# Attention of a fused kernel rewritten in unit slots: V and ones stationary, softmax weights moving, operands stacked by DMAs, convolution on VectorE

## What is computed

```python
# attention: a key counts only where the 6-bit hash of q and k agrees
q_bits = (q @ proj) > 0; k_bits = (k @ proj) > 0      # buckets of 6 bits
mask = q_bucket[:, None] == k_bucket[None, :]
scores = where(mask, scale * q @ k.T, -1e9)
attn = exp(scores - max(scores)); attn /= sum(attn) + 1e-9
x = attn @ v                                          # 16 heads of 768x768
# gated convolution
gate = sigmoid(causal depthwise convolution of x, 5 taps)
y = (gate * (x @ w_val)) @ w_out
# Fourier mixing and feed-forward
u = y + real(fft(fft(y, axis=1), axis=2))
out = u + relu(norm(u) @ w_ch1) @ w_ch2
```

## Time and profile before

| what | value |
|---|---|
| device time, median of 3 runs | 797.1 us (795.99 to 800.96) |
| span of the profiled execution | 798.6 us |
| PE busy | 746.9 us, 94% |
| PEld busy | 704.5 us, 88% |
| DVE busy | 389.7 us, 49% |
| ACT busy | 271.1 us, 34% |
| POOL busy | 352.6 us, 44% |
| DMA | 29.13 MB, mean 36 GB/s |

### The profile page before, as it was taken

One profiled execution on the slowest core, in us unless ns is written; L12 is line 12 of the kernel. 1 busy time (PEld: TensorE's weight loads), 2 busy tenths in 40 slices (PEclk: granted clock), 3 DMA queues, 4 the chain that ended last, 5 costly groups with the idle time before them and its releaser, 6 DMA issues.

```text
span 798.6 us, 12617 instructions
## 1 busy us (share of the span) xinstructions
PE 746.9 (94%) x4358; PEld 704.5 (88%) x4358; DVE 389.7 (49%) x680; ACT 271.1 (34%) x489; POOL 352.6 (44%) x334
## 2 busy tenths in 40 slices
PE   3898989899898889989999999999999999999998
PEld 2898988899798889989989899999999989999997
DVE  6655666655655765664476457953222212122112
ACT  4353534545245554524643343411111111111110
POOL 1237475574756657474987579578300000000000
PEclk9798978979889998979999999999999999999999
DMA  6010111111011111001012111333010001001001
GB/s 151 12 47 10 38 47 47 46 46 26 20 46 46 46 46 46 17 1 32 1 37 57 34 53 41 93 87 99 27 39 0 0 0 39 0 0 40 0 1 40
DMA packets 27938, 29.13 MB, mean 36 GB/s; under 512 B 14848, under 2 KB 19200, under 8 KB 27904
## 3 DMA queue, kind: packets, MB, share of 16 engines
q1 hardware_dynamic: 27904, 28.68, 13.0%
HBM read 25.52 MB, written 3.15 MB: 36 GB/s over the span
## 4 chain that ended last, share of the span: by engine, by line
PE 75%; DVE 13%; issue 5%; POOL 4%; ACT 1%; DMA 0%; SPq 0%; DVEq 0%; ACTq 0%; POOLq 0%
PE psum L1031 63%; PE psum L1082 9%; DVE a2k L770 3%; DVE a1q L768 3%; DVE max_half L783 2%; DVE den L806 2%; POOL taps L464 1%; ACT probs L599 1%; PE psum L1098 1%; PE psum L1107 1%; PE psum L1229 1%; DVE neg_parts L794 1%; DMA k_raw<-in_k 0%; PE psum L1088 0%; DVE neg_rest L796 0%
## 5 line engine op out<-in xcount | busy, mean ns | idle before, releaser
L1082 PEld LDWEIGHTS psum<-va,probs 128*128 128x128 f32 x1152 | 153.9, 205 | 6.0 <-ACT probs L599 4.3
L1082 PE MATMUL psum<-va,probs 128*128 128x65 f32 x1152 | 152.6, 284 | 3.2 <-ACT probs L599 3.2
L783 DVE TENSOR_REDUCE max_half<-psum 128x1 f32<-128x384 f32 x192 | 97.0, 551 | 82.0 <-PE psum L1031 79.8
L599 ACT ACTIVATE probs<-psum 128x384 f32<-128x384 f32 x192 | 86.0, 490 | 134.6 <-PE psum L1031 132.9
L1002 DVE SCALAR_TENSOR_TENSOR h_lo<-psum,h_hi 128x384 fp32r<-128x384 f32 x64 | 35.7, 558 | 183.3 <-ACT h_hi L749 183.3
L749 ACT ACTIVATE h_hi<-psum 128x384 fp32r<-128x384 f32 x64 | 31.5, 492 | 215.4 <-PE psum L1031 215.4
L1031 PE MATMUL psum<-a1k,a1q 128*128 128x384 f32 x192 | 78.9, 411 | 23.2 <-DVE max_half L783 20.2
L1031 PE MATMUL psum<-unt_hi,w_hi 128*128 (+1 forms) x256 | 86.9, 339 | 0.0
L1031 PE MATMUL psum<-unt_lo,w_hi 128*128 (+1 forms) x256 | 86.3, 337 | 0.0
L1031 PE MATMUL psum<-unt_hi,w_lo 128*128 (+1 forms) x256 | 85.9, 336 | 0.0
L1031 PE MATMUL psum<-a1q,a1k 128*128 128x384 f32 x192 | 75.1, 391 | 2.1 <-DVE a2q L777 1.9
(11 more groups left out here) (132 smaller groups left out, 1446.9 us busy)
## 6 DMA issues: line engine op xcount, KB each, us to landing
stg_w<-in_w SPq DMA_DIRECT2D x32, 256.0 KB, 2.6
k_raw<-in_k SPq DMA_DIRECT2D x32, 192.0 KB, 3.6
q_raw<-in_q SPq DMA_DIRECT2D x16, 192.0 KB, 3.3
va<-in_v SPq DMA_DIRECT2D x16, 192.0 KB, 3.1
out<-y SPq DMA_DIRECT2D x12, 256.0 KB, 2.1
stg_b<-in_w_b SPq DMA_DIRECT2D x16, 137.0 KB, 2.1
stg_a<-in_w_a SPq DMA_DIRECT2D x16, 128.0 KB, 2.7
proj_raw<-in_proj SPq DMA_DIRECT2D x1, 128.0 KB, 2.1
```

Of the source, the lines that this page charges most:

```text
L599: act.activation(probs[:, at_:at_ + HALF], psum[:, ST_BANKS[m % 2], 0:HALF], ACT.Exp, scale=SCALE).then_inc(exp_done, 1)
L783: dve.tensor_reduce(max_half[:, m:m + 1], psum[:, S_BANKS[m % 3], 0:HALF], AX.X, ALU.max).then_inc(max_done, 1)
L1082: mm = pe.matmul(psum[:, PV_BANK, t * DV:(t + 1) * DV], probs[:, at_:at_ + P], va3[par][:, j, :], start=(j == 0 and t == 0), stop=(j == T ...
```

## The change

All engines now follow one list of unit slots g, from -20 to 95 (and a few behind it), written out with no loop. A slot is one tile of 128 keys or queries with all 768 columns. On TensorE, slot g holds the turned scores of unit g+2, the scores of unit g+10, and `weigh_v` of unit g. Six slots are a head, twelve a pair.

- **`weigh_v`** loads the 128x128 block `v1` (64 columns of V, 64 of ones) as the weight and moves the 768 columns of `probs` past it in two float32 matmuls, of 384 and 385 columns. The result is already channels by queries, with the row sums beside it. The 385th column, of ones, gives the sum of all V, so L1088, `sum_v` and `turn_x` are gone.
- **`scores`** has one pair of banks instead of three single ones: it waits for the maximum of the unit directly before. `maximum` takes 768 columns in one instruction.
- **Stacking.** ScalarE and VectorE make hi and lo of q and k together (`hi_qk`, `lo_qk`, one instruction of 128x768 each per head), and six DMAs per head (`stack`) copy them from SBUF to SBUF into `a1q`, `a1k`, `a2q`, `a2k`. Hash bits of a pair of heads are made by one instruction and stacked by four DMAs (`stack_bits`). The hash of a pair is 12 matmuls at slot 10 of 12.
- **Rows of one number per query** are spread over partitions through memory: a flag row (no match) is stored and loaded back to 128 partitions (`spread_flag`), the denominators go to 128x6 (`fold_den`), their reciprocals are stored and loaded back to 64 partitions (`spread_rec`). Where a load follows a store, SP itself waits for the store.
- **VectorE** adds the flag's share and evacuates PSUM (`take_sums`) and computes the whole convolution, one instruction of 768 columns per tap. **GpSimd** keeps `split_weights` and multiplies with the reciprocal (`scale_x`).

```diff
-                for t in tiles:
-                    at_ = (j % 3) * S + t * P
-                    mm = pe.matmul(psum[:, PV_BANK, t * DV:(t + 1) * DV], probs[:, at_:at_ + P], va3[par][:, j, :],
-                                   start=(j == 0 and t == 0), stop=(j == T - 1), skip_group_check=True)
...
+                if j == 0:
+                    pe.wait_ge(v_loaded[par], 16 * (n // 2 + 1))
+                    if n > 0:
+                        pe.wait_ge(sums_ready, n)
+                pe.wait_ge(probs_ready, i + 1)
+                pe.matmul(first, v1[par][:, w], probs[i % PBUF][:, 0:HALF], start=j == 0, stop=j == T - 1)
+                pe.matmul(last, v1[par][:, w], probs[i % PBUF][:, HALF:PCOLS], start=j == 0, stop=j == T - 1).then_inc(pv_done, 1)
...
+            for g in range(FIRST, UNITS):
+                pair, n = g // (2 * T), g // T
+                if g % T == 3 and 0 <= n + 1 < NH:
+                    turn_max(n + 1)
+                if 0 <= g + ST_LEAD < UNITS:
+                    turned_scores(g + ST_LEAD)
+                if 0 <= g + S_LEAD < UNITS:
+                    scores(g + S_LEAD)
+                if g % (2 * T) == 10 and 0 <= pair + 2 < NPAIR:
+                    hash_pair(pair + 2)
+                if 0 <= g:
+                    weigh_v(g)
```

On SP (`stack` has two more copies of lo behind a wait for `qk_lo_ready`):

```diff
+                sp.dma_start(bits(a1q[s][0:D, :]), hi[0:D, :]).then_inc(set_loaded[s], 16)
+                sp.dma_start(bits(a1k[s][0:D, :]), hi[D:P, :]).then_inc(set_loaded[s], 16)
+                sp.dma_start(bits(a1k[s][D:P, :]), hi[D:P, :]).then_inc(set_loaded[s], 16)
+                sp.dma_start(bits(a2q[s][0:D, :]), hi[0:D, :]).then_inc(set_loaded[s], 16)
...
+                sp.wait_ge(max_rows, n + 1)
+                sp.dma_start(flag_dram[n:n + 1, :], bits(a2q[n % SETS][FLAG:FLAG + 1, :])).then_inc(flag_stored, 16)
+                if n >= 2:
+                    sp.wait_ge(sums_ready, n - 1)
+                sp.wait_ge(flag_stored, 16 * (n + 1))
+                sp.dma_start(flag_b[n % 2][:, :], flag_dram[n:n + 1, :].to_broadcast([P, S])).then_inc(flag_loaded[n % 2], 16)
...
+                if g % (2 * T) == 10 and 0 <= pair + 3 < NPAIR and pair + 3 >= RAWS // 2:
+                    load_qk(2 * (pair + 3))
+                    load_qk(2 * (pair + 3) + 1)
+                if g % (2 * T) == 6 and 0 <= pair + 2 < NPAIR:
+                    stack(2 * (pair + 2))
+                if g % (2 * T) == 10 and 0 <= pair + 2 < NPAIR:
+                    stack(2 * (pair + 2) + 1)
+                if g % (2 * T) == 0 and 0 <= pair + 1 < NPAIR:
+                    stack_bits(pair + 1)
```

More of the change, by code:

```diff
@@ L502, in fold_tile @@
+            for g in range(FIRST, UNITS + T):
+                n = g // T
+                if g % T == 1 and 0 <= n < NH:
+                    split_weights(n)
+                if g % T == 4 and 1 <= n <= NH:
+                    scale_x(n - 1)
+                    pool.wait_ge(x_ready, n)
             def fold_tile(b, f):
@@ new lines, in lo_x @@
+            def lo_x(b, c):
+                at_ = (CT * b + c) * S
+                dve.wait_ge(x_hi_ready, CT * b + c + 1)
+                dve.tensor_tensor(x_lo[:, c * S:(c + 1) * S], xT[:, at_:at_ + S], bits(x_hi[:, c * S:(c + 1) * S]), ALU.subtract).then_inc(x_lo_ready, 1)
+            dve.wait_ge(conv_loaded, 16)
+            for g in range(FIRST, UNITS):
+                pair, n = g // (2 * T), g // T
+                if g % T == 0 and 1 <= n:
+                    take_sums(n - 1)
+                if 0 <= g + S_LEAD < UNITS:
+                    maximum(g + S_LEAD)
+                if g % T == 1 and 0 <= n + 1 < NH:
+                    max_parts(n + 1)
+                if g % (2 * T) == 10 and 0 <= pair + 2 < NPAIR:
+                    sign_bits(pair + 2)
+                if g % (2 * T) == 5 and 0 <= pair + 2 < NPAIR:
+                    lo_qk(2 * (pair + 2))
+                if g % (2 * T) == 7 and 0 <= pair + 2 < NPAIR:
+                    lo_qk(2 * (pair + 2) + 1)
+                if g % T == 2 and 1 <= n:
+                    reciprocals(n - 1)
+                slot, tap = (g - 18) // (2 * T), (g - 18) % (2 * T) // 2
+                if 0 <= slot < NPAIR - 1 and (g - 18) % 2 == 0 and tap < KCONV:
+                    convolve(slot, tap)
+                if g - 1 in X_SLOTS:
+                    lo_x(0, X_SLOTS.index(g - 1))
@@ L874, in lo_gv @@
+            take_sums(NH - 1)
             def lo_gv(n):
@@ L1027, in _, with product @@
         def _(pe):
-            def product(dst, pairs, done=None, first=True, last=True, skip=False):
+            def product(dst, pairs, done=None, first=True, last=True):
                 for n, (lhs, rhs) in enumerate(pairs):
-                    mm = pe.matmul(dst, lhs, rhs, start=first and n == 0, stop=last and n == len(pairs) - 1,
-                                   skip_group_check=skip)
+                    mm = pe.matmul(dst, lhs, rhs, start=first and n == 0, stop=last and n == len(pairs) - 1)
@@ L1092, in turn_max @@
-            def turn_max(n, xs, prepared):
-                pe.wait_ge(max_step, 3 * (n + 1))
-                pe.wait_ge(qbits_ready, prepared)
-                pe.wait_ge(x_ready, xs)
+                    for m in range(2):
+                        n, w = 2 * pair + m, slice(m * P, (m + 1) * P)
+                        hi, lo = qk_hi[n % 2][:, cols], qk_lo[n % RAWS][:, cols]
+                        product(ring[use % 2][:, half, :], [(ph_hi[:, w], hi), (ph_hi[:, w], lo), (ph_lo[:, w], hi)],
+                                done=hashed if half and m else None, first=m == 0, last=m == 1)
@@ new lines, in scores @@
+            def scores(i):
+                n, t = i // T, i % T
+                s, rows = n % SETS, slice(t * P, (t + 1) * P)
+                if t == 0:
+                    pe.wait_ge(set_loaded[s], 128 * (n // SETS + 1))
+                if i > 0:
+                    pe.wait_ge(max_done, i)
+                for half in range(2):
+                    cols = slice(half * HALF, (half + 1) * HALF)
+                    product(s_ps[:, half, :], [(a1q[s][:, rows], a1k[s][:, cols]), (a2q[s][0:MX, rows], a2k[s][0:MX, cols])],
+                            done=s_done if half else None)
```

792 lines of the change are left out of this document (333 added, 459 removed).

## The result

| | before | changed kernel |
|---|---|---|
| device time, median | 799.0 us (796.0 to 806.1) | 870.1 us (867.7 to 877.3) |
| ratio to before | | 1.090, 95% interval 1.083 to 1.097 |
| profiled span | 798.6 us | 875.5 us |
| first `weigh_v` | 31.1 us | 53.5 us |
| last head ends | 392.2 us | 471.9 us |

The change made the kernel 9% slower, where 6% faster was forecast. Each ratio in this document is to executions of the kernel before taken beside it, whose medians lie between 797.7 and 800.1 us, so a difference of 2 us between kernels of different sections says little. The first view is that of the stretches of the changed kernel, columns as in the earlier trace rows: start, attention from the first `weigh_v` to its last, and the rest.

What follows compares the result with a forecast made beforehand. TensorE's work, waits and slow clock were taken as the bound. Start 53, work 290.6, `take_sums` 1.6 and late bits 3.5 made 349 against 392.2; with 1.5 saved behind, 752 us, range 735 to 790.

Steps and rivals of the forecast that it cites:

- the bullet on SP: SP's DMA list per pair: 32 issues 19 us, four store waits of 2.1 us, data 25.6 of 38.1 us.
- the tight chain: From slot 8 through reciprocals, loads, stacking and flag row to hash bits: 0.2 us late, 3.5 us taken for 7 pairs.
- The bound and its causes: Attention before: 290 us TensorE work, 75 us waits and slow clock; VectorE late, its instructions slow while GpSimd is busy.
- The price of the wide `weigh_v`: On TensorE, each new slot's `weigh_v`: 1.53 us against 1.35, with three unhidden weight loads, 0.16.
- the change of kind behind it: On TensorE, the matmul kind changes behind `weigh_v`: 0.09 us per slot.
- the lower bound of 1.37: On TensorE, `weigh_v` per slot if nothing is unhidden: 1.37 us; upper bound 1.81.
- The case that I gave 0.15: Rival on TensorE: `weigh_v` weight loads are hidden because wide records leave time; total 742; chance 0.15.
- The start: Loads, copies, then single-buffered scores before attention: first `weigh_v` at 53 us against 31.1, bounds 47 and 58.
- VectorE's queue: VectorE in attention: 21 us of 38 per pair, maxima have slack, slow subtractions mostly become 0.95 us.
- `take_sums` and `turn_max`: Between heads on TensorE: `take_sums` 0.1 us late each, 1.6 in all; `turn_max` 0.43 us each, 15 make 6.5.
- The clock: TensorE in attention: near 1.00 from about 55 us; rival that it stays at 0.89, total 789, chance 0.10.
- The slower rival: Copies in the hash-bits chain at 120 GB/s: 10 us late a pair, total 828; chance 0.07.

Runs made afterwards that it cites:

- the edit to the start: Against the kernel copying bits before the flag row: loads for heads 2, 3 (q, k) and 0, 1 (V, weights) issued behind the first copies; 729.4 us, ratio 0.912.

## Why the prediction was wrong

**The step that failed** is the bullet on SP. It counted issues, bytes and store round trips, and it wrote the tight chain out from the reciprocals at 26.9 us, as if SP were free then. The load of V that stands ahead of them in the same slot is one of its 32 issues, but its wait for `pv_done` is in no term. The wait is not met in slot 8 of the pair: the buffer that V goes to is read until slot 11. So SP reaches the store of the reciprocals not at 26.9 but behind the pair, at 35.4 and more (12 slots of 2.70, 2.1 for the hash, 0.86 for `turn_max`). With that one number the same chain gives the changed kernel: 18.0 us from the store of the reciprocals to the bits' arrival in the prediction (26.9 to 44.9); here V goes out at 209.56 and the store at 210.88, and 19.4 us later, at 230.31, TensorE starts. The same wait stands in slot 2, for which the prediction had no chain at all. What the runs showed in place of "0.2 late": 13 us a pair for the bits, 205 us of SP standing at this load, and 131 us of device time back when it is asked for one head later. The rows of SP quoted in the change begin three rows too late; the first of the three carries the answer:

```text
L360 DMA v_1_104<-in_v 128x6x64 [waits pv_done]
L366 DMA stg_a<-in_w_a 128x256 [waits wa_split]
L410 DMA rec_dram<-rec_c 128x6 [waits rec_ready]
L414 DMA rec_b<-rec_dram 64x768 [waits rec_stored0,x_ready]
```

The other terms of the chain held, but partly by luck. Without the wait the bits cost 3.2 us in the steady part, where 3.5 were taken, though a pair became 2.8 us shorter than forecast (12 times 0.23) and the copies faster than the 211 GB/s taken (277 in the stretch shown).

**The bound and its causes: right.** That attention before lost 75 us to waits and to the slow clock, that VectorE was the releaser and GpSimd's convolution what slowed it: the kernel with the convolution alone moved shows each link, and gives back 58 of them. The sum was 5 us short (30 of waits and 40 of slow clock make 70 of the 75), and that kernel says why: busy 298.6 us at a clock of 0.99, its work is nearer to 296 than to 290.

**The price of the wide `weigh_v`: too high.** 1.30 us (2.70 less eight times 0.175), not 1.53. Four times per column is right (0.65 us for the two records of L1085, 208.07 to 208.72). The unhidden weight loads are not: the records are 0.32 us apart, which is their 768 columns at 2.4 GHz and nothing more. Nor are the 0.09 for the change of kind behind it, so 1.30 lies even below the lower bound of 1.37. The case that I gave 0.15, hidden loads, is what the trace of the changed kernel shows. The Trainium skill, TensorE: Matmul & The Clock Gate, Part 2, says that weight loads are pulled ahead of matmuls in flight; these rows agree, at 0.32 us a record. The records of 65 columns are 0.11 us apart where their columns take 0.054; that the rest is an unhidden load stays inferred from its size. The mis-sized term is 96 x 0.23 = 22 us.

**The start: right**, 53 forecast, 53.5 measured, and in its parts: the first scores start at 24.07 us (24.6 forecast) and stand 2.70 us apart (2.55). 5.9 us of it were data, as the edit to the start showed. Matmuls stand 0.32 us apart there, up to 48.8 us, which is 1.2 GHz as forecast, although the clock column of the stretch reads 1.00. The distance of starts is the better witness at the start of a profile.

**VectorE's queue: right; `take_sums` and `turn_max`: too low.** In the kernel with V one head ahead no row of TensorE waiting for a maximum is left behind 60 us. But a slot with `turn_max` takes 3.33 us there and not 2.70, 0.63 where 0.43 was taken, and the first `weigh_v` of an odd head starts 0.35 late where 0.1 was taken. The slot with `turn_max`:

```profile
206.51 0.81 PE L1086 MATMUL psum<-probs,v 128*128 128x384 f32 x2
...
207.90 0.50 PE L1072 MATMUL psum<-ident_b,neg_parts 128*4 128x128 bf16 x6
...
209.84 0.81 PE L1086 MATMUL psum<-probs,v 128*128 128x384 f32 x2
```

**The clock: half right.** It is 1.00 in attention without the wait. In the changed kernel it is 0.85, and the slow rows stand behind idle stretches of TensorE, as the prediction read before the change: behind the idle 14.64 us that end at 230.31 the matmuls start 0.32 us apart, 384 columns at 1.2 GHz.

```profile
230.79 0.52 PE L1010 MATMUL psum<-a2k,a2q 96*128 96x384 f32 x1
231.11 0.52 PE L1010 MATMUL psum<-a1k,a1q 128*128 128x384 f32 x1
```

This is a consequence of the waits and not a rival of its own, since taking the wait away brings 1.00. Of the 137 us by which the stretch of attention is longer than without the wait (418.5 against 281.4), 105 are more idle time (111 less 6) and 32 are the same matmuls at a slower clock (307.2 us busy against 275.4).

**The slower rival** had the right place, the copies of hash bits, and the wrong cause, their rate. The total alone would have spoken for its price of 10 us a pair at 120 GB/s; halving the bytes and removing the wait tell them apart. With the missing wait put right, the forecast is 13 us from the measured 739.0, or 16 by the profiled spans (754 and 737.7): 22 for `weigh_v`, against it 8, about 1 us a pair, for the gaps around `turn_max` and `take_sums`, and 1.6 from the start and the end.

## What to carry to other kernels

On an engine that issues DMAs in order, take every wait in its list, in order, and ask at what time it is met; a prefetch that asks for a buffer which is still being read stops everything queued behind it. The earliest useful place for such a load is where the buffer comes free, and its cost elsewhere is not its bytes but the length of the list behind it. When a large rewrite comes out slower, do its parts alone: here one part in the old kernel and one moved load in the new one give the same 739 us, the first without the rest of the rewrite.

## What the runs showed of the hardware

- A float32 matmul of 384 columns against a 128x128 weight costs two records 0.322 us apart at full clock, which is what its columns take; one of 65 columns costs 0.11 us per record, twice what its columns take. So six narrow matmuls (1.26 us) cost nearly as much as two wide ones (1.30), though they move half of the columns.
- VectorE's subtraction of 64x768 float32 takes 0.95 us with no GpSimd instruction beside it, and 2.10 to 2.47 beside GpSimd's multiply and add of the convolution. The 128x6 instruction `den` takes 0.16 us in one case and 1.76 in the other. What stands beside an instruction tells more than GpSimd's busy share: at 36% busy and never beside them, the subtractions kept their 0.95. It is no strict rule: one of L768 before, at 177.65 us, has the same convolution rows beside it and takes 0.95. Moving 39 us of work (the rows of L825 and L828 between 50 and 340 us) onto the engine that others wait for left it busy for 17 us less in attention.
- A store of one 3 KB row, whose landing SP waits for, held SP for 3.8 us from its issue at 221.15, behind two loads of q with k and six copies, and for 1.5 us in the kernel with V one head ahead (188.00 to 189.46), where SP had issued nothing for 5 us. The view of DMA issues of the changed kernel gives the median to landing:

```profile
rec_dram<-rec_c SPq DMA_DIRECT2D x16, 3.0 KB, 2.2
```
